# Who makes the low halves of the first layer's weights: VectorE or GpSimd

## The chip, the cores and the metric

One core of a Trainium2 chip runs the kernel. The metric is the device time of one execution in microseconds. TensorE, VectorE (DVE in the rows), ScalarE (ACT), GpSimd (POOL) and the DMA queue of SyncE (SP) each run their own list of instructions in order, and meet through semaphores.

## The reference

Four batches of eight heads, 768 steps, head size 48: a linear attention whose state is a matrix per head that turns and decays by a complex gate per key channel; then two MLP layers over 3072 tokens of width 384 with 2048 hidden units. The first has a leaky ReLU, the second an ELU.

```python
for t in range(S):
    new_re = ar * S_re - ai * S_im          # ar, ai: gate of step t, clipped to 0.999
    new_im = ar * S_im + ai * S_re
    S_re, S_im = new_re + outer(k[t], v[t]), new_im
    y[t] = q[t] @ S_re
h = x @ w_in;  g = maximum(0.01 * h, h);                 x = g @ w_out      # layer 1
h = x @ w_in2; g = where(h > 0, h, exp(minimum(h, 0)) - 1); out = g @ w_out2 # layer 2
```

## The kernel before

The attention is done in 24 chunks of 128 steps (6 per batch, batches interleaved). The first MLP layer starts on the first two chunks while the later ones are still computed; its seven tiles have 2, 3, 4, 4, 4, 4 and 3 chunks. The second layer has six tiles of 512 tokens. Each tile is 16 items: `up(n)` (L866) multiplies the tile by one strip of `w_in` of 128 hidden units, the activation is made by ScalarE (L366) and VectorE (L562), and `down(n)` (L886) multiplies by the strip of `w_out`.

Every matrix product of the MLP is made of three: a float32 operand is split in a high half, rounded to `fp32r`, and a low half, the rest. TensorE adds hi x hi, hi x lo and lo x hi. For the weights this split is made once per layer and strip. A strip is 128 x 768 numbers: 384 columns of `w_in` and 384 of `w_out`. There are 16 strips per layer (`FC`), n = 0 to 15 for the first. SyncE loads strip n into one of two raw buffers `wraw` (`WS = 2`) with four DMAs (L275, L279); ScalarE casts it to the high half (L356, semaphore `w_hi`); VectorE subtracts the high half from the raw strip (L553, semaphore `w_lo`). The load of strip n waits for the low half of strip n - 2 to be done, since it reuses that raw buffer. `up(n)` of the first tile waits for the low half of strip n.

The order of work on each engine is one loop over numbered slots, `for a in SLOTS`. In each slot an engine issues what falls due there: items of the MLP every 64 slots, steps of attention chunks every 256, and for the first eight chunks and the first layer's 16 strips the slots that are written out as lists. `weights_at(a, 0, lead)` gives the strips of the first layer whose entry in the list `lead` equals `a`, and those of the second layer by a formula. Since every engine takes its list in order, an instruction that waits holds up all behind it on that engine.

Steps of a chunk that the text names:
- L603, L604, L608, L412 to L418, L623: squares, their sum, the gain of the gate. L898 on TensorE turns the gain over to channels; L632 is its running product, L918 turns it back.
- L616 to L618, L433: the angle. L906 sums angles on TensorE for the first chunks; L658 to L660 bring the sum into one turn (L650 is a running sum for the later ones).
- L451 to L455, L467 to L470 on ScalarE: roots, sines and cosines. L679 to L683 scale q and k on VectorE, L706 and L707 turn them. L948 turns them over to channels on TensorE, L483 copies them out on ScalarE, L956 makes the scores, L714 masks them, L971 and L980 make y, L491 and L746 split y into the high and low half of x.
- L571 is the low half of the activation.

GpSimd makes constants at the start, masks and an identity, and then has no work.

Of the kernel before, what the change touches and what calls it, by code (L numbers as in the profile page):

```python
# [6 lines left out]
F32 = mybir.dt.float32  # L7
F32R = mybir.dt.float32r
ALU = mybir.AluOpType
# [16 lines left out]
def fused(nc, sem, q, k, v, a_re, a_im, weights, out, hidden, weak, attention, mlps):  # L26
# [9 lines left out]
    KC, FC = E // P, F // P  # L36
    FIRST, START, PACE, LEAD = -100122, 848, 64, 8
    WLAG, XSTEP, WS, TB = 3, 4, 2, TOK // P
# [16 lines left out]
    def chunks_at(a, offset, lead=()):  # L55
        m, r = divmod(a - START - offset, 4 * PACE)
        return [c for c, x in enumerate(lead) if x == a] + ([m + LEAD] if r == 0 and 0 <= m < M - LEAD else [])
# [5 lines left out]
    def first(m):  # L63
        return m < B

    def end(m):
        return m >= M - B
# [7 lines left out]
    with ExitStack() as ctx:  # L75
        def sb(name, shape, dt=F32):
            return ctx.enter_context(nc.sbuf_tensor(name, shape, dt))
# [4 lines left out]
        ws = [sb(f"w_{n}", [P, FC, 2, E], F32R) for n in ("hi", "lo")]  # L82
        wraw = sb("wraw", [P, WS, 2, E])
# [107 lines left out]
        w_hi, w_lo = sem("w_hi"), sem("w_lo")  # L191
# [19 lines left out]
        def weights_at(a, ahead, lead):  # L211
            j, r = divmod(a + ahead - PACE * ((T1 - 1) * FC + WLAG), PACE)
            return [i for i, x in enumerate(lead) if x == a] + ([FC + j] if r == 0 and 0 <= j < FC else [])
# [326 lines left out]
        def _(dve):  # L540
# [57 lines left out]
            def square_sum(m):  # L598
                x = sq_of(m)
                if m < 2:  # L600
                    dve.wait_ge(in_re[m], 16)
                    dve.wait_ge(in_im[m], 16)
                    step(vec.tensor_tensor(x, gate[:, m], gate[:, m], ALU.mult))  # L603
                    vec.scalar_tensor_tensor(x[:, 0], x[:, 0], 0.0, x[:, 1], ALU.add, ALU.add,  # L604
                                             accum_out=sizes[:, m:m + 1]).then_inc(sq_sum, 1)
                else:
                    dve.wait_ge(squares, m - 1)
                    vec.tensor_tensor(x[:, 0], x[:, 0], x[:, 1], ALU.add).then_inc(sq_sum, 1)  # L608
# [100 lines left out]
            def mask(m):  # L709
                if used(m):  # L710
                    dve.wait_ge(y_made, used(m))
                for half, bank in enumerate(halves(m)):
                    dve.wait_ge(scores_made, 2 * m + half + 1)
                    vec.tensor_tensor(scm_of(m)[:, 4 * half:4 * half + 4], split(bank[:], 4),  # L714
                                      causal[:].unsqueeze(1).broadcast_to([P, 4, P]), ALU.mult).then_inc(masked, 1)
# [41 lines left out]
            def verdict():  # L757
                dve.wait_ge(worst_t, 1)
                vec.tensor_reduce(worstrow[:, 0:1], chain[0:1, 0:2 * P], mybir.AxisListType.X, ALU.min)
                step(vec.tensor_reduce(worstrow[:, 1:2], chain[0:1, 2 * P:2 * P + D2], mybir.AxisListType.X, ALU.min))  # L760
                step(vec.tensor_scalar(worstrow[:, 1:2], worstrow[:, 1:2], WEAK, None, ALU.is_ge))
                step(vec.tensor_tensor(flags[:], worstrow[:, 0:1], worstrow[:, 1:2], ALU.mult))
                vec.tensor_scalar(weak[:], flags[:], 0.5, None, ALU.is_lt).then_inc(judged, 1)

            dve.wait_ge(const_ready, 10)
            for a in SLOTS:
                if a == JUDGE + 2 * PACE:
                    verdict()
                for m in chunks_at(a, 864, (-136, -136, -71, 147, 498, 765, 1204, 1396)):
                    mask(m)  # L770
                for m in chunks_at(a, 292, (-451, -451, -298, -171, -109, 51, 456, 781)):
                    square_sum(m)
                for m in chunks_at(a, 377, (-393, -349, -240, -128, -9, 181, 569, 834)):
                    gains(m)
                for m in chunks_at(a, 663, (-205, -157, -135, -32, 279, 659, 915, 1252)):
                    ends_out(m)
                for m in chunks_at(a, 976, (-138, -115, -17, 301, 564, 899, 1233, 1438)):
                    if not end(m):
                        sum_state(m)
                if (n := item_at(a, 18)) is not None:  # L780
                    split_g(n)
                if a == JUDGE:
                    judge()
                for m in chunks_at(a, 545, (-307, -291, -204, -109, 92, 402, 712, 1122)):
                    phases(m)
                if (T := finished_at(a)) is not None:
                    if T < len(tiles) - 1:
                        result(T)
                    else:
                        last_result()  # L790
                for m in chunks_at(a, 440, (-362, -324, -211, -119, 14, 359, 697, 1036)):
                    decays(m)
                for m in chunks_at(a, 1053, (-100122, -100056, -100001, -99969, 594, 1013, 1356, 1592)):
                    if not first(m) and not end(m):
                        next_state(m)
                for m in chunks_at(a, 367, (-450, -368, -283, -200, -75, 162, 453, 867)):
                    tangents(m)
                for m in chunks_at(a, 697, (-214, -200, -129, 13, 250, 682, 991, 1315)):
                    turns(m)
                if (x := x_step_at(a)) is not None:  # L800
                    split_x(*x)
                for n in weights_at(a, 0, (-326, -210, -169, -168, -122, -36, 47, 73, 246, 249, 380, 414, 516, 530, 703, 752)):
                    split_w(n)
                for m in chunks_at(a, 562, (-216, -215, -159, -61, 232, 509, 795, 1230)):
                    scale_by_decay(m)
                for m in chunks_at(a, 985, (-121, -120, 31, 296, 666, 890, 1282, 1530)):
                    chunk_to_x(m)
                for m in chunks_at(a, 602, (-306, -290, -185, -48, 206, 443, 828, 1231)):
                    ends(m)
                if (n := item_at(a, 82)) is not None:  # L810
                    from_h(n)
# [8 lines left out]
        @block.gpsimd  # L820
        def _(pool):
            gp = nc.gpsimd
            gp.memset(vs[:, 0], 0.0)
            gp.memset(vs[:, 1], 0.0).then_inc(pads_ready, 1)
            gp.memset(ident[:], 0.0).then_inc(pool_chain, 1)
            gp.memset(causal[:], 1.0).then_inc(pool_chain, 1)
            gp.memset(pick[:], 0.0).then_inc(pool_chain, 1)
            gp.memset(member[:], 1.0).then_inc(pool_chain, 1)
            pool.wait_ge(pool_chain, 4)
            gp.affine_select(out=ident[:], in_=ident[:], compare_op=ALU.not_equal, fill=1.0, base=0,  # L830
                             pattern=[[-1, P]], channel_multiplier=1).then_inc(const_ready, 1)
            gp.affine_select(out=causal[:], in_=causal[:], compare_op=ALU.is_ge, fill=0.0, base=0,
                             pattern=[[1, P]], channel_multiplier=-1).then_inc(const_ready, 1)
            gp.affine_select(out=member[:, 0], in_=member[:, 0], compare_op=ALU.is_ge, fill=0.0, base=D - 1,
                             pattern=[[0, HP]], channel_multiplier=-1).then_inc(const_ready, 1)
            gp.affine_select(out=member[:, 1], in_=member[:, 1], compare_op=ALU.is_ge, fill=0.0, base=-D,
                             pattern=[[0, HP]], channel_multiplier=1).then_inc(const_ready, 1)
            gp.affine_select(out=pick[:], in_=pick[:], compare_op=ALU.not_equal, fill=-0.5, base=0,
                             pattern=[[0, 2], [-1, D]], channel_multiplier=1).then_inc(pool_chain, 1)
            pool.wait_ge(pool_chain, 5)  # L840
            gp.affine_select(out=pick[:], in_=pick[:], compare_op=ALU.not_equal, fill=-0.5, base=-D,
                             pattern=[[0, 2], [-1, D]], channel_multiplier=1).then_inc(const_ready, 1)
            gp.memset(ones[:], 1.0).then_inc(const_ready, 1)
            gp.memset(lneps[:], math.log(MAG_EPS)).then_inc(const_ready, 1)
            gp.memset(half[:], -0.5).then_inc(const_ready, 1)
            gp.memset(rest[:], 0.75).then_inc(const_ready, 1)
            gp.memset(endmin[:], 1.0).then_inc(const_ready, 1)


        @block.tensor  # L850
# [605 lines left out]
```

## Time and profile before

| what | value |
|---|---|
| median of three runs | 1046.76 us (1046.31 to 1048.47) |
| profiled execution, its own time | 1047.74 us |
| its span | 1046.0 us |
| TensorE busy | 1010.8 us (97%), 6926 matmuls |
| VectorE busy | 680.1 us (65%) |
| ScalarE busy | 575.9 us (55%) |
| GpSimd busy | 3.2 us, 21 instructions |
| DMA | 51.57 MB, mean 49 GB/s |

The span is what the trace covers; the time of an execution holds a little more around it. Busy shares over the whole span hide that the first tenth is another kind of work than the rest, so the windows by stage say more than this table. Matmul ends are modelled in the trace.

### The profile page before, as it was taken

To read this page: it belongs to the slowest core of one execution; us is meant where nothing else is said; L and a number is where in the kernel's file an instruction comes from. 1 tells how busy PE (TensorE), PEld (TensorE's weight loads), DVE (VectorE), ACT (ScalarE), POOL (GpSimd) and SP (SyncE) were. 2 spreads that over 40 slices of the span, in tenths; PEclk is the share of its full clock that TensorE was granted. 3 is DMA by queue.
4 is the path that set the end of the run, shared out by engine and by line. 5 is a ranking of instruction groups with operands and counts; after the bars stand their busy time and mean duration, and the time that the engine had idled before them with its cause. 6 is when DMAs were issued, how large, how long until landed. Compare 5 with 4: busy or idle time off the path is not lost.

```text
span 1046.0 us, 17995 instructions
## 1 busy us (share of the span) xinstructions
PE 1010.8 (97%) x6926; PEld 907.4 (87%) x6926; DVE 680.1 (65%) x1361; ACT 575.9 (55%) x1089; POOL 3.2 (0%) x21
## 2 busy tenths in 40 slices
PE   2889999999999999999999999999999999999998
PEld 1779999988888888888888999999999999999997
DVE  7999988887777777777753376445445444454443
ACT  8988877776666667666643365323333233333332
POOL 1000000000000000000000000000000000000000
PEclk8899999999999999999999999999999999999999
DMA  7564343222222232223200244001010010010000
GB/s 151 105 121 101 70 54 78 45 39 39 61 39 39 39 69 39 38 40 76 54 1 1 79 133 144 1 1 61 1 53 9 1 61 1 16 46 1 31 1 34
DMA packets 176044, 51.57 MB, mean 49 GB/s; under 512 B 151504, under 2 KB 172112, under 8 KB 175952
## 3 DMA queue, kind: packets, MB, share of 16 engines
q1 hardware_dynamic: 175952, 50.35, 22.4%
q8 instruction: 57, 0.93, 0.4%
q14 instruction: 35, 0.29, 0.1%
HBM read 40.89 MB, written 9.44 MB: 48 GB/s over the span
## 4 chain that ended last, share of the span: by engine, by line
PE 91%; DVE 5%; issue 1%; ACT 1%; DMA 1%; SPq 0%; ACTq 0%; DVEq 0%
PE ph L866 37%; PE acc L886 33%; PE even L886 5%; PE odd L996 2%; PE even L948 2%; PE odd L948 2%; PE even L956 2%; PE odd L956 2%; PE even L971 1%; PE chain L898 1%; PE even L980 1%; PE even L975 1%; PE even L984 1%; PE chain L918 1%; DMA wraw<-in_moe_w_out 1%
## 5 line engine op out<-in xcount | busy, mean ns | idle before, releaser
L374 ACT CAST g_hi<-gf 128x512 fp32r<-128x512 f32 (+2 forms) x208 | 122.4, 588 | 219.0 <-PE even L886 128.9
L866 PE MATMUL ph<-x_hi,w_lo 128*128 128x512 f32 (+2 forms) x624 | 235.1, 377 | 0.0
L866 PE MATMUL ph<-x_lo,w_hi 128*128 128x512 f32 (+2 forms) x624 | 234.6, 376 | 0.0
L866 PE MATMUL ph<-x_hi,w_hi 128*128 128x512 f32 (+2 forms) x624 | 233.6, 374 | 0.0
L366 ACT ACTIVATE gx<-ph 128x512 f32<-128x512 f32 (+2 forms) x208 | 117.8, 566 | 157.2 <-PE ph L866 156.7
L571 DVE TENSOR_TENSOR g_lo<-gf,g_hi 128x512 fp32r<-128x512 f32 (+2 forms) x208 | 134.6, 647 | 105.3 <-ACT g_hi L374 104.1
L866 PEld LDWEIGHTS ph<-x_hi,w_lo 128*128 128x128 f32 x624 | 117.6, 188 | 19.2
L866 PEld LDWEIGHTS ph<-x_lo,w_hi 128*128 128x128 f32 x624 | 117.7, 189 | 16.8
L866 PEld LDWEIGHTS ph<-x_hi,w_hi 128*128 128x128 f32 x624 | 117.8, 189 | 16.2
L886 PE MATMUL acc<-g_hi,w_hi 128*128 128x512 f32 (+2 forms) x336 | 128.8, 383 | 0.3 <-DVE g_lo L571 0.2
L886 PE MATMUL acc<-g_hi,w_lo 128*128 128x512 f32 (+2 forms) x336 | 121.3, 361 | 0.0
L886 PE MATMUL acc<-g_lo,w_hi 128*128 128x512 f32 (+2 forms) x336 | 120.9, 360 | 0.0
L564 DVE TENSOR_SCALAR gx<-gx 128x512 f32<-128x512 f32 x96 | 41.1, 428 | 121.1 <-ACT gx L366 121.1
L886 PE MATMUL acc<-w_lo,g_hi 128*128 128x384 f32 x288 | 97.5, 338 | 0.0
L886 PE MATMUL acc<-w_hi,g_hi 128*128 128x384 f32 x288 | 97.2, 338 | 0.0
L886 PE MATMUL acc<-w_hi,g_lo 128*128 128x384 f32 x288 | 96.9, 336 | 0.0
L562 DVE TENSOR_TENSOR gf<-ph,gx 128x512 f32<-128x512 f32 (+2 forms) x112 | 68.0, 607 | 19.9 <-ACT gx L366 19.8
L886 PEld LDWEIGHTS acc<-g_hi,w_lo 128*128 128x128 f32 x336 | 63.1, 188 | 8.3
L886 PEld LDWEIGHTS acc<-g_hi,w_hi 128*128 128x128 f32 x336 | 63.4, 189 | 7.3 <-issue 0.8
L886 PEld LDWEIGHTS acc<-g_lo,w_hi 128*128 128x128 f32 x336 | 63.5, 189 | 5.9
L566 DVE SCALAR_TENSOR_TENSOR gf<-ph,gx 128x512 f32<-128x512 f32 x96 | 66.4, 692 | 3.3
L348 ACT ACT_TABLE_LOAD x49 | 62.9, 1283 | 1.6 <-PEq L1446 0.8
(216 smaller groups left out, 1541.3 us busy)
## 6 DMA issues: line engine op xcount, KB each, us to landing
wraw<-in_moe_w_out SPq DMA_DIRECT2D x32, 192.0 KB
gate<-in_a_re SPq DMA_DIRECT2D x24, 192.0 KB, 4.1
gate<-in_a_im SPq DMA_DIRECT2D x24, 192.0 KB, 4.1
qk<-in_q SPq DMA_DIRECT2D x24, 192.0 KB, 3.1
qk<-in_k SPq DMA_DIRECT2D x24, 192.0 KB, 3.7
rot<-hidden SPq DMA_DIRECT2D x6, 768.0 KB, 5.8
out<-res SPq DMA_DIRECT2D x5, 768.0 KB, 4.3
wraw<-in_moe_w_in SPq DMA_DIRECT2D x48, 64.0 KB
```

The lines of the kernel that those rows point to most:

```text
L348: act.preload_act_table_set(name)
L366: sc.activation(gx[:, n % 2, 0:size], ph[n % 2][:, 0:size], ACT.Exp if layer else ACT.Copy, scale=1.0 if layer else 0.01).then_inc(h_act, 1)
L374: sc.copy(gs[0][:, n % 2, 0:size], gf[:, n % 2, 0:size]).then_inc(g_hi, 1)
L562: vec.tensor_tensor(fb, hb, xb, ALU.max).then_inc(g_full, 1)
L564: vec.tensor_scalar(xb, xb, 1.0, -1.0, ALU.min, ALU.add).then_inc(e_ready, 1)
L566: vec.scalar_tensor_tensor(fb, hb, 0.0, xb, ALU.max, ALU.add).then_inc(g_full, 1)
L571: vec.tensor_tensor(gs[1][:, n % 2, 0:size], gf[:, n % 2, 0:size], gs[0][:, n % 2, 0:size].bitcast(F32), ALU.subtract).then_inc(g_lo, 1)
L866: ins = mm(ph[n % 2][:, 0:size], ws[hi][:, j, 0, kc * P:(kc + 1) * P], xs[lo][:, T % 2, kc, 0:size], start=i == 0, stop=i == KC * len(PART ...
L886: ins = mm(o, lhs, rhs, start=j == 0 and i == 0, stop=j == FC - 1 and i == 2)
L948: ins = tr(bank[0:D2, h * P:(h + 1) * P], rot[:, i, 4 * half + h].rearrange("p r d -> p (r d)"), ident[:])
L956: ins = mm(bank[:, (h % 4) * P:(h % 4 + 1) * P], k_of(m)[:, h], q_of(m)[:, h], start=True, stop=True)
L996: ins = mm(sum_bank(m)[0:D2, h * DP:(h + 1) * DP], rot[:, 1, h].rearrange("p r d -> p (r d)"), vs[:, m % 2, h], start=True, stop=True)
```

## The change

The list of slots for the first layer's strips on VectorE becomes empty, so VectorE makes low halves only for the second layer. GpSimd, behind its constants, loops over the 16 strips of the first layer, waits for each high half and makes the low half by the same subtraction into the same tile. The casts on ScalarE, the loads on SyncE with their slots, and TensorE's waits are as they were.

```diff
@@ VectorE @@
-                for n in weights_at(a, 0, (-326, -210, -169, -168, -122, -36, 47, 73, 246, 249, 380, 414, 516, 530, 703, 752)):
+                for n in weights_at(a, 0, ()):
                     split_w(n)
@@ GpSimd @@
             gp.memset(endmin[:], 1.0).then_inc(const_ready, 1)
+            for n in range(FC):
+                pool.wait_ge(w_hi, n + 1)
+                gp.tensor_tensor(ws[1][:, n], wraw[:, n % WS], ws[0][:, n].bitcast(F32), ALU.subtract).then_inc(w_lo, 1)
```

## Rows read from the trace of the kernel before

**Rows 1.** Windows: start, end, length, each engine's busy us, PEclk, DMA share, GB/s.

```profile
10.00:50.00 40.00, 25.27 (x217) 21.59 (x218) 37.20 (x85) 37.42 (x70) 0.00 (x0) 0.83 0.70 131
50.00:84.00 34.00, 28.48 (x275) 26.00 (x274) 31.45 (x74) 29.59 (x61) 0.00 (x0) 0.95 0.56 109
84.00:125.00 41.00, 40.20 (x443) 39.19 (x443) 39.22 (x90) 35.77 (x77) 0.00 (x0) 1.00 0.45 102
125.00:440.00 315.00, 315.00 (x2567) 280.32 (x2566) 251.39 (x547) 225.14 (x445) 0.00 (x0) 1.00 0.29 48
```

**Rows 2.** Waits of TensorE from 84 us on: total us, times, longest.

```profile
PE chain L929 <- DVE qk L683: 0.5, 1, 0.5
PE acc L886 <- DVE g_lo L571: 0.2, 1, 0.2
```

**Rows 3.** Groups by line, first 130 us: count, busy us, mean ns, idle before.

```profile
L553 DVE TENSOR_TENSOR w_lo<-wraw,w_hi 128x768 fp32r<-128x768 f32 x16 | 15.0, 946 | 0.6 <-ACT w_hi L356 0.5
```

**Rows 4.** Timeline of VectorE: start us, duration us, instruction, idle before it.

```profile
5.05 0.96 DVE L603 TENSOR_TENSOR sq<-gate 128x768 f32<-128x768 f32 x1 [5.05 <-DMA gate<-in_a_im]
...
13.14 0.53 DVE L623 SCALAR_TENSOR_TENSOR res<-res 128x384 f32<-128x384 f32 x1
...
14.86 1.36 DVE L632 TENSOR_TENSOR_SCAN gx<-acc,ones 96x128 f32<-96x128 f32 x4 [0.31 <-PE acc L898]
...
18.90 0.55 DVE L608 TENSOR_TENSOR sq<-sq 128x384 f32<-128x384 f32 x1
...
29.63 0.95 DVE L707 TENSOR_TENSOR rot<-roots,qk 128x768 f32<-128x768 f32 x1
...
33.89 0.56 DVE L658 TENSOR_SCALAR turn<-chain 128x384 f32<-128x384 f32 x1 [1.05 <-PE chain L906]
...
39.70 1.81 DVE L553 TENSOR_TENSOR w_lo<-wraw,w_hi 128x768 fp32r<-128x768 f32 x2
41.44 0.55 DVE L679 TENSOR_TENSOR sines<-chain,sines 128x384 f32<-128x384 f32 x1
...
47.35 0.94 DVE L706 SCALAR_TENSOR_TENSOR rot<-sines,qk 128x768 f32<-128x768 f32 x1
...
55.49 0.56 DVE L658 TENSOR_SCALAR turn<-chain 128x384 f32<-128x384 f32 x1 [1.75 <-PE chain L906]
...
117.38 0.95 DVE L553 TENSOR_TENSOR w_lo<-wraw,w_hi 128x768 fp32r<-128x768 f32 x1
```

**Rows 5.** Timeline of ScalarE: casts of strips 0, 1 and 15, and one L470.

```profile
11.81 0.81 ACT L356 CAST w_hi<-wraw 128x768 fp32r<-128x768 f32 x1
...
27.97 0.82 ACT L356 CAST w_hi<-wraw 128x768 fp32r<-128x768 f32 x1
...
46.33 0.51 ACT L470 ACTIVATE sines<-sines 128x384 f32<-128x384 f32 x1
...
115.45 0.84 ACT L356 CAST w_hi<-wraw 128x768 fp32r<-128x768 f32 x1
```

**Rows 6.** Timeline of GpSimd: three pairs of neighbours.

```profile
0.80 0.52 POOL L823 MEMSET vs<- 128x512 f32 x1 [0.29 <-POOLq L1446]
1.26 0.52 POOL L824 MEMSET vs<- 128x512 f32 x1
1.73 0.20 POOL L825 MEMSET ident<- 128x128 f32 x1
1.87 0.20 POOL L826 MEMSET causal<- 128x128 f32 x1
...
2.46 0.29 POOL L830 TENSOR_SCALAR_AFFINE_SELECT ident<-ident 128x128 f32<-128x128 f32 x1 [0.23 <-POOL member L828]
2.71 0.29 POOL L832 TENSOR_SCALAR_AFFINE_SELECT causal<-causal 128x128 f32<-128x128 f32 x1
```

**Rows 7.** Waits of SyncE's queue, first 125 us: total us, times, longest.

```profile
SPq L275 <- DVE w_lo L553: 28.3, 6, 7.8
```

**Rows 8.** Timeline of TensorE: the first matmul of `up(15)` in the first tile.

```profile
119.02 0.29 PE L866 MATMUL ph<-x_hi,w_hi 128*128 128x256 f32 x1
```

## Prediction

> **What bounds the kernel now.** I read the windows by stage first. From 125 us on TensorE is busy without a gap at full clock (315 of 315 us), and from 84 to 125 us nearly so; before that it is busy 25.3 of 40 us (10 to 50) and 28.5 of 34 us (50 to 84), at a mean granted clock of 0.83 and 0.95 (part of it at 1.2 in place of 2.4 GHz) [rows 1]. The reader should see that only the first 84 us have TensorE time to win or lose in bulk. TensorE's waits after 84 us say the same: two waits, 0.7 us in total, both on VectorE [rows 2]. In those first 84 us two engines are nearly full: VectorE 37.2 of 40 and 31.5 of 34 us, ScalarE 37.4 of 40 and 29.6 of 34 us [rows 1]. The order on every engine is written out by hand and fixed, so whoever is late there makes TensorE late, and a delay at 84 us is a delay of the end. The timelines of VectorE and ScalarE are read next, around the slots of the strips.
>
> **What leaves VectorE.** The 16 subtractions that make the low halves of the first layer's strips: 16 x 0.946 us busy = 15.1 us, all within the first 130 us [rows 3]. Two in a row take 1.81 us, less an overlap of 0.07 at the next start; from start to start one takes 0.87 us (39.70 for two, and the next instruction at 41.44) [rows 4]. I use 0.87. Ten of the 16 (strips 0 to 9) run before 84 us, the last one at 117.38 [rows 4]. The code of the second layer's 16 is as it was.
>
> What those ten are worth, if nothing else changes:
> - Strips 0 and 1 give nothing. Behind the first one VectorE still waits 0.31 us for TensorE, whose transpose needs the L623 at 13.14, ahead of the subtraction; behind the second it waits 1.05 us for the cumulative sum of the angles [rows 4].
> - Strips 2 and 3 (39.70) free 1.74 us, but the L706 at 47.35 needs ScalarE's L470, which starts at 46.33 and ends at 46.84 [rows 4, 5]. So 0.5 us is left.
> - Strip 4 gives 0.8 us more: the low halves of x come right behind it, then TensorE's transposes and first layer product, and the 1.75 us that VectorE waits at 55.49 is for them, so it moves along [rows 4]. That is 1.3 us.
> - Strips 5 to 9 give some 0.2 us in all: there the scaling steps wait for ScalarE's roots, or VectorE for TensorE. Total at 84 us: 1.5 us.
> - Behind 84 us TensorE can win back at most its 0.7 us of idle [rows 2]. The total is -2.2 us. Its bounds are 0 and 8 x 0.87 = 7.0 us; ScalarE's idle time from 50 to 84 us, 34 - 29.6 = 4.4 us [rows 1], makes more than about 4.5 us implausible.
>
> **What arrives on GpSimd.** 16 subtractions 128x768 with two inputs in SBUF. The trace has no such instruction on GpSimd. From start to start a MEMSET of 512 columns takes 0.46 us and one of 128 takes 0.14 us, so 0.83 ns per column written; an AFFINE_SELECT (one input) of 128 columns takes 0.25 us, some 1.7 ns per column [rows 6]. For 768 columns that is 0.64 us from the one, 1.35 us from the other; with a second input read at 0.83 ns per column 2.0 us. Ends: 0.7 and 2.0 us. I take 1.7 us, by the AFFINE_SELECT, which also reads, plus part of the second input. In a sentence that the sum does not need: the Trainium skill (GPSIMD Engine Reference, "Elementwise — side-by-side cycle accounting") gives 4497 ns for a two-input operation on 2048 columns, by which an estimate for 768 is 1.7 us; no row here shows it.
>
> GpSimd's queue holds nothing else once its 21 small instructions are over (3.2 us busy; none from 10 us on [rows 1]), so nothing stands behind a waiting subtraction. It starts when the high half is there, so the low half comes about 1.8 us after ScalarE's cast ends. Before, VectorE came to strip 15 at 117.38 on a cast that ended at 116.29 [rows 4, 5], and SyncE's 28.3 us of waiting for low halves [rows 7] shows that others came later still, so most low halves now come earlier. The buffers get free earlier too. Earlier loads win little, since TensorE has only the 0.7 us to win behind 84 us. No load, cast or matmul is added or moved in its queue.
>
> **The disputed cost: two engines reading SBUF together.** After the change GpSimd works 16 x 1.7 = 27 us inside a stretch where VectorE is full. The trace shows no overlap of the two: GpSimd is busy 3.2 us at the very start and never from 10 us on, and VectorE's first instruction starts at 5.05, behind a DMA [rows 1, 4]. What a row shows is that VectorE reads two SBUF operands at once: the L608 with two SBUF inputs takes 0.55 us for 384 columns, and the L658 with one input in PSUM 0.56 us [rows 4]. Bounds: the two engines do not disturb each other (0), or one stands still for the whole instruction of the other whenever both want two SBUF operands. With the hold, by strips:
> - Strip 0: the cast (11.81, 0.81) ends at 12.62 [rows 5]; GpSimd runs from 12.7 to 14.4. The scan before 13.2 reads one SBUF operand and goes on; the L623 of 13.14 waits to 14.4: +1.3 us. TensorE's idle transpose and the scan at 14.86 follow it [rows 4].
> - Strip 1: the cast (27.97, 0.82) ends at 28.79 [rows 5], when VectorE is in the first of the two rotations (L706, L707), both with two SBUF inputs. The second, at 29.63, waits: +1.7 us. TensorE waits for it. Subtotal +3.0 us.
> - Strips 2 and 3 (their casts move with the delay so far): the first falls on a scan and a wait for TensorE, 0; the second takes about 1.2 us out of the 1.74 freed, net -0.5 us. Subtotal +2.5 us.
> - Strips 4 to 9: one (strip 7) falls on a scan. Five holds of 1.7 = 8.5 us against six removed instructions of 0.87 = 5.2 us: +3.3 us. Together +5.8 us.
> - Some of it lands where ScalarE is last (strips 5 to 9 above, where time won by VectorE gave almost nothing); I take off 0.8 us. Total +5.0 us.
> - Strips 10 to 15 at 0: six holds of 1.7 = 10.2 us at most, of which some six tenths meet two-input work, against 5.2 us removed and 1.8 us of idle (41 - 39.2) [rows 1].
>
> With a GpSimd instruction of 1.35 us the same steps give 0.9 + 1.35 - 0.9 + 1.6 = +3.0 us, with 2.0 us +8 us. I cannot choose between hold and no hold by rows; the choice is a judgement. For the hold speaks that VectorE uses two SBUF reads a cycle and that the added work needs two as well. By the Trainium skill (SBUF — State Buffer, "Who interferes with whom") a VectorE instruction with two SBUF inputs contends with a GpSimd instruction that reads SBUF, and the one that comes second is blocked until the first is done: by that rule +5.0 us, without it -2.2 us; no row of this trace shows which.
>
> **Forecast and rivals**, against the median of 1046.76 us. The profiled execution's own time is 1047.74 us (span 1046.0), 1.0 us above the median, so 1052.7 us by that execution is 1051.8 us by the median. The measurement tells about 0.2% (2.1 us) from no change.
> - **Forecast: hold.** GpSimd's reads stop VectorE's two-input instructions in the first 84 us: +5.0 us, 1051.8 us; own range 1049.5 to 1055. Chance 0.52.
> - **Rival 1: no disturbance.** VectorE is relieved and ScalarE takes over as the bound: -2.2 us, 1044.6 us (1043 to 1046). Chance 0.32. For it: GpSimd is empty and the slack of every strip is there. Against it: nothing in the trace has both engines at work. It decides if VectorE's instructions keep their durations beside GpSimd's.
> - **Rival 2: partial.** Either instruction is only stretched, or GpSimd is the one that waits most of the time. The break-even is where a strip's subtraction costs VectorE as much as it frees: 0.87 us for strips 2 to 9, and nothing for 0 and 1. With half of each hold, 0.65 + 0.85 - 1.1 + (4.25 - 5.2) = -0.5 us: 1046.2 us. Chance 0.13.
> - **Rival 3: low halves too late.** The last strip is the tightest: cast 115.45 + 0.84 = 116.29, low half by GpSimd at 118.1, by VectorE at 118.3 before; TensorE wants it at 119.02 [rows 4, 5, 8]. Only with over 2.6 us per instruction would it wait, and then by tenths: 1047.5 us. Chance 0.03.
>
> Chances: faster by over 0.2% 0.18 (a little over half of rival 1), within 0.2% 0.29, slower 0.53. Range: from rival 1's 1044.0 to 1054.5 us, which leaves out the lowest part of rival 1 and the top of the hold.
>
> **What would show it.** The profile after has 16 subtractions on POOL of 1.3 to 2 us from the cast's end, no L553 on VectorE in the first 125 us. If the hold is right, VectorE's two-input forms (L623, L707, L618, L682) have single instructions of 1.5 to 2.5 us in the first 120 us, or idle gaps in front of them beside a GpSimd instruction, and VectorE's L623 for chunk 1 ends near 15 us instead of 13.7. TensorE's last product with strip 15 in the first tile, now at 119.02 [rows 8], comes 5 us later. If those durations are as before and that product comes 2 us earlier, rival 1 is right. The prediction is wrong if the two engines read side by side, or if GpSimd's instruction is much longer than 2 us.

## The result: 12 us slower

The changed kernel takes 1059.66 us (median of five, 1057.57 to 1061.35); the kernel before took 1048.47 us on the same chip (1046.31 to 1049.33). The ratio, taken from the means of the two sets of five, is 1.0114, 95% interval 1.0093 to 1.0134; so the loss is 11.2 us by the medians and 11.9 us by the means. The direction was forecast, the size was not: 1051.8 us with a range to 1054.5 us stood on record. The profiled execution took 1059.66 us; its span is 1057.9 us, 11.9 us over the span of 1046.0 us before.

The timeline of GpSimd in the changed kernel has the 16 subtractions, each started by ScalarE's cast. Four of them:

```profile
12.90 1.80 POOL L850 TENSOR_TENSOR w_lo<-wraw,w_hi 128x768 fp32r<-128x768 f32 x1 [8.71 <-ACT w_hi L356]
30.30 2.51 POOL L850 TENSOR_TENSOR w_lo<-wraw,w_hi 128x768 fp32r<-128x768 f32 x1 [15.60 <-ACT w_hi L356]
...
51.04 1.85 POOL L850 TENSOR_TENSOR w_lo<-wraw,w_hi 128x768 fp32r<-128x768 f32 x1 [6.22 <-ACT w_hi L356]
...
69.39 3.59 POOL L850 TENSOR_TENSOR w_lo<-wraw,w_hi 128x768 fp32r<-128x768 f32 x1 [7.29 <-ACT w_hi L356]
```

One takes 1.80 us where it runs at once, against VectorE's 0.946 us [rows 3], and the slowest, 3.59 us, had to wait itself. The answer to rows 4 is in the timeline of VectorE. Every line but the L632 is an instruction that took 0.16 to 0.95 us before:

```profile
13.30 1.81 DVE L623 SCALAR_TENSOR_TENSOR res<-res 128x384 f32<-128x384 f32 x1
16.30 1.36 DVE L632 TENSOR_TENSOR_SCAN gx<-acc,ones 96x128 f32<-96x128 f32 x4 [1.18 <-PE acc L901]
...
31.07 2.56 DVE L707 TENSOR_TENSOR rot<-roots,qk 128x768 f32<-128x768 f32 x1
...
43.54 1.69 DVE L680 SCALAR_TENSOR_TENSOR sines<-sines,roots 128x384 f32<-128x384 f32 x1
...
51.15 2.56 DVE L707 TENSOR_TENSOR rot<-roots,qk 128x768 f32<-128x768 f32 x1
...
60.44 2.08 DVE L618 SCALAR_TENSOR_TENSOR ang<-inv,ang 128x384 f32<-128x384 f32 x1
...
75.90 1.86 DVE L659 TENSOR_SCALAR turn<-turn 128x384 f32<-128x384 f32 x1
...
82.89 1.88 DVE L623 SCALAR_TENSOR_TENSOR sq<-sq 128x384 f32<-128x384 f32 x1
...
85.14 1.74 DVE L671 SCALAR_TENSOR_TENSOR endmag<-rootd,parted 96x8 f32<-96x8 f32 x1
...
98.50 1.87 DVE L571 TENSOR_TENSOR g_lo<-gf,g_hi 128x256 fp32r<-128x256 f32 x1 [0.35 <-ACT g_hi L374]
...
102.34 1.95 DVE L659 TENSOR_SCALAR turn<-turn 128x384 f32<-128x384 f32 x1
...
107.13 2.19 DVE L618 SCALAR_TENSOR_TENSOR ang<-inv,ang 128x384 f32<-128x384 f32 x1
...
127.62 2.03 DVE L571 TENSOR_TENSOR g_lo<-gf,g_hi 128x256 fp32r<-128x256 f32 x1
```

Read two timelines side by side here. The L623 at 13.30 starts while GpSimd's first subtraction runs (12.90 to 14.70) and ends 0.4 us after it. The L632 is a scan with no GpSimd instruction beside it; it keeps its 1.36 us and only comes late, behind TensorE. The L671 handles 8 columns, took 0.16 us before and takes 1.74 us: the time is not the instruction's own, it ends when GpSimd does. The other 12 instructions and the L623 at 116.07 (0.89 us) are longer by 18.2 us in all than the same instructions in the kernel before, by 0.35 to 1.63 us each; what was taken off VectorE is 16 x 0.87 = 13.9 us. Instructions with an operand in PSUM kept their times: L679 (it reads `chain`) and L562 (it reads `ph`) beside GpSimd at 42.96 and 82.56 took 0.55 and 0.42 us, as before.

The windows of the changed kernel, with the stretches of [rows 1], and after them TensorE from the first matmul of `up(6)` to that of `up(16)`, first after, then before (in a fence of its own):

```profile
10.00:50.00 40.00, 23.69 (x178) 20.82 (x182) 35.35 (x78) 34.39 (x66) 7.93 (x4) 0.79 0.67 126
50.00:84.00 34.00, 26.99 (x297) 24.61 (x286) 32.14 (x63) 29.82 (x62) 11.23 (x5) 0.95 0.59 114
84.00:125.00 41.00, 34.88 (x326) 34.11 (x325) 34.38 (x68) 29.00 (x61) 11.31 (x7) 0.92 0.42 99
125.00:440.00 315.00, 314.36 (x2643) 280.80 (x2642) 253.35 (x551) 225.44 (x447) 2.04 (x1) 1.00 0.30 49
92.55:136.46 43.91, 40.77 (x433) 39.66 (x432) 38.88 (x82) 34.38 (x73) 11.19 (x6) 0.95 0.37 77
```

```profile
84.97:124.61 39.64, 38.84 (x434) 37.83 (x433) 37.86 (x88) 34.41 (x75) 0.00 (x0) 1.00 0.47 106
```

`up(6)` starts at 92.55 in place of 84.97 (+7.6 us), `up(16)` at 136.46 in place of 124.61 (+11.9 us), and the span is 11.9 us longer: nothing more is lost or won behind it. So 7.6 us come from the stage that the forecast had at +5.0, and 4.3 us from the stage that it had at 0. In that last stage TensorE's idle time went from 0.8 to 3.1 us, and its busy time for the same work from 38.8 to 40.8 us, at a mean granted clock of 0.95 in place of 1.00. Of TensorE's waits from 10 to 140 us in the changed kernel these five grew most, all on what the held instructions make or pass on (GpSimd's loop moves TensorE's lines by three: L901 is L898 of the kernel before, L932 is L929, L951 is L948, L889 is L886). Before, in this order, they were 12.8, 1.6, 1.8, 2.1 and 0.2 us:

```profile
PE chain L901 <- DVE sq L623: 14.7, 3, 10.7
PE chain L932 <- DVE qk L683: 3.6, 1, 3.6
PE even L951 <- DVE rot L707: 3.4, 1, 3.4
PE acc L901 <- DVE res L623: 3.4, 1, 3.4
PE acc L889 <- DVE g_lo L571: 3.1, 3, 2.2
```

### The profile page after: what moved, and what is told of

Its sections match the earlier page's. It is cut to its first block, busy times and chain, and to the rows that moved or that the text cites. A ratio compares the mean times of both kernels' runs of the same rounds, so it can differ in the third digit from the quotient of the medians.

```text
span 1057.9 us, 17995 instructions
## 1 busy us (share of the span) xinstructions
PE 1013.6 (96%) x6926; PEld 910.9 (86%) x6926; DVE 685.1 (65%) x1345; ACT 576.0 (54%) x1089; POOL 35.7 (3%) x37
## 4 chain that ended last, share of the span: by engine, by line
PE 91%; DVE 5%; ACT 2%; issue 1%; DMA 0%; SPq 0%; DVEq 0%; ACTq 0%
PE ph L869 37%; PE acc L889 33%; PE even L889 5%; PE odd L999 2%; PE even L951 2%; PE odd L951 2%; PE even L959 2%; PE odd L959 2%; PE even L974 1%; PE chain L901 1%; PE even L983 1%; PE even L978 1%; PE even L987 1%; PE chain L932 1%; PE chain L921 1%
## 5 line engine op out<-in xcount | busy, mean ns | idle before, releaser
L571 DVE TENSOR_TENSOR g_lo<-gf,g_hi 128x512 fp32r<-128x512 f32 (+2 forms) x208 | 137.6, 662 | 105.3 <-ACT g_hi L374 104.1
L889 PE MATMUL acc<-g_hi,w_hi 128*128 128x512 f32 (+2 forms) x336 | 129.9, 387 | 3.1 <-DVE g_lo L571 3.1
L889 PE MATMUL acc<-g_hi,w_lo 128*128 128x512 f32 (+2 forms) x336 | 122.5, 365 | 0.0
L889 PE MATMUL acc<-g_lo,w_hi 128*128 128x512 f32 (+2 forms) x336 | 122.0, 363 | 0.0
L889 PE MATMUL acc<-w_lo,g_hi 128*128 128x384 f32 x288 | 97.5, 338 | 0.0
L889 PE MATMUL acc<-w_hi,g_hi 128*128 128x384 f32 x288 | 97.2, 338 | 0.0
L889 PE MATMUL acc<-w_hi,g_lo 128*128 128x384 f32 x288 | 96.9, 336 | 0.0
L562 DVE TENSOR_TENSOR gf<-ph,gx 128x512 f32<-128x512 f32 (+2 forms) x112 | 68.0, 608 | 19.3 <-ACT gx L366 19.3
L889 PEld LDWEIGHTS acc<-g_hi,w_hi 128*128 128x128 f32 x336 | 64.5, 192 | 10.4 <-DVE g_lo L571 3.8
L889 PEld LDWEIGHTS acc<-g_hi,w_lo 128*128 128x128 f32 x336 | 64.4, 192 | 8.3
L889 PEld LDWEIGHTS acc<-g_lo,w_hi 128*128 128x128 f32 x336 | 64.6, 192 | 5.9
```

Source lines behind the costliest of these rows:

```text
L562: vec.tensor_tensor(fb, hb, xb, ALU.max).then_inc(g_full, 1)
L571: vec.tensor_tensor(gs[1][:, n % 2, 0:size], gf[:, n % 2, 0:size], gs[0][:, n % 2, 0:size].bitcast(F32), ALU.subtract).then_inc(g_lo, 1)
L889: ins = mm(o, lhs, rhs, start=j == 0 and i == 0, stop=j == FC - 1 and i == 2)
```

## The experiments

**Is it GpSimd's reading?** Two theories: A, GpSimd's reads of SBUF stop VectorE; C, nothing is stopped, but low halves and loads come at other times and upset the hand-written order. In the first kernel GpSimd only writes (a MEMSET to zero; the first layer's low halves are left out):

```diff
-                gp.tensor_tensor(ws[1][:, n], wraw[:, n % WS], ws[0][:, n].bitcast(F32), ALU.subtract).then_inc(w_lo, 1)
+                gp.memset(ws[1][:, n].bitcast(F32), 0.0).then_inc(w_lo, 1)
```

> GpSimd's 16 instructions of the first layer only write: each sets its strip's low half to zero (128x768, no input), at the same place and behind the same waits, so the low halves of the first layer are left out of the result. Theory A (GpSimd's reads stop VectorE's instructions): nothing is read, so L623 of chunk 1 is back at 0.53 us, L707 at 0.95 us, and only the relief is left: 2 us faster than the kernel before, 1045 us. Theory B (any GpSimd instruction that touches SBUF stops VectorE, writes too): each holds for its own 0.7 us, about +2 us. Theory C (the order of the queues is upset once VectorE is not the one that makes low halves, whatever GpSimd does): still some +8 to +12 us.

Measured: 1043.71 us against 1046.72 us, ratio 0.9971 (0.9962 to 0.9981): 3.0 us faster. GpSimd's first MEMSET runs beside the same L623 that was held before, and the L623 does not mind. Timelines of GpSimd and VectorE in this kernel:

```profile
12.81 0.74 POOL L850 MEMSET w_lo<- 128x768 f32 x1 [8.61 <-ACT w_hi L356]
...
68.84 0.74 POOL L850 MEMSET w_lo<- 128x768 f32 x1 [3.91 <-ACT w_hi L356]
```

```profile
13.27 0.53 DVE L623 SCALAR_TENSOR_TENSOR res<-res 128x384 f32<-128x384 f32 x1
...
69.02 0.77 DVE L658 TENSOR_SCALAR turn<-phase 128x384 f32<-128x384 f32 x1
```

So C is wrong where it says that the loss comes with the move itself, and the relief is real: 3.0 us. The second line of VectorE is the one exception among the instructions beside a MEMSET: a one-input instruction from SBUF to SBUF that takes 0.36 us elsewhere took 0.77 us beside a MEMSET.

In the second kernel the work is only added: VectorE keeps all its subtractions, GpSimd repeats those of strips 0 to 13.

```diff
+                    sp.wait_ge(p_lo, min(n - WS + 1, FC - 2))       # SyncE, load n
+                if n == FC - 1:                                     # VectorE, split_w
+                    dve.wait_ge(p_lo, FC - 2)
+            for n in range(FC - 2):                                 # GpSimd
+                pool.wait_ge(w_hi, n + 1)
+                pool.wait_ge(p_lo, n)
+                gp.tensor_tensor(ws[1][:, FC - 1], wraw[:, n % WS], ws[0][:, n].bitcast(F32), ALU.subtract).then_inc(p_lo, 1)
```

> VectorE makes all low halves as in the kernel before; GpSimd makes those of strips 0 to 13 a second time, at the times of the changed kernel, into the place of strip 15's low half, which VectorE overwrites at the end. Work is only added, none taken away, and no low half is late. Theory A (reads hold VectorE): fourteen holds of 1.8 us with no relief; the loss is that of the changed kernel or more, +11 to +18 us, with instructions of 1.7 to 2.6 us on VectorE. Theory C (lateness or order, no hold): within 1 us of the kernel before.

Measured: 1063.98 us against 1046.72 us, ratio 1.0172 (1.0155 to 1.0189): +17.3 us. GpSimd's added work costs this much, with VectorE's own work and order as before. A raw buffer is also held until GpSimd has read it, but in this trace no cast of the first layer waits for its load. The loss is about what the changed kernel lost plus the relief that it got (12 + 3 = 15 us). VectorE's own subtractions have two SBUF inputs too, and two of the 16 are held (2.57 and 2.59 us in place of 0.95). All that is longer on VectorE sums to 15.4 us, not more than the 18.2 us of the changed kernel, so where the 2 us above 15 come from stays open.

**Which strips?** Strips 0 to 9 by GpSimd and the rest by VectorE in the old slots, and the other way about (the list of slots with `None` for GpSimd's strips, GpSimd's loop over its own, and a wait on `w_lo` where one engine follows the other).

```diff
-                for n in weights_at(a, 0, ()):
+                for n in weights_at(a, 0, (None, None, None, None, None, None, None, None, None, None, 380, 414, 516, 530, 703, 752)):
-            for n in range(FC):
+            for n in (0, 1, 2, 3, 4, 5, 6, 7, 8, 9):
                 pool.wait_ge(w_hi, n + 1)
+                pool.wait_ge(w_lo, n)
```

> Strips 0 to 9 by GpSimd, 10 to 15 by VectorE in their old slots. The stage up to 84 us of the kernel before is as in the changed kernel, that behind it has no hold. If the forecast's split were right, all the loss is here: +12 us. If the holds of strips 10 to 15 cost as the trace of the changed kernel says (the delay grows from 6.4 us at the L683 of 82.65 to 11.7 us at that of 122.09), this one loses 6 to 8 us.

> Strips 0 to 9 by VectorE in their old slots, 10 to 15 by GpSimd. If late strips cost nothing, as the forecast said (six holds against the removed work and VectorE's idle time): within 1 us of the kernel before. If their holds fall on instructions that TensorE waits for (L571, L618): +3 to +5 us, and the sum of this one and of the one with strips 0 to 9 is about the changed kernel's +11 us.

Measured: strips 0 to 9 cost 1056.02 us, ratio 1.0085 (1.0063 to 1.0106), +9.3 us by the medians; strips 10 to 15 cost 1050.48 us, ratio 1.0039 (1.0025 to 1.0053), +3.8 us. The sum of 13 us is the changed kernel's loss within the intervals. Six late strips, expected to be covered, are a quarter to a third of the loss. Their mechanism shows in TensorE's waits from 84 to 140 us of the kernel with strips 10 to 15, where before there were 0.2 us on L571 [rows 2] (L573 is L571 and L892 is L886 in the lines of this kernel):

```profile
PE acc L892 <- DVE g_lo L573: 3.4, 3, 2.2
```

**How much of it is the second input, how much the length?** GpSimd copies the raw strip (one input; the low halves hold the raw weights), and GpSimd subtracts in four pieces of 192 columns:

```diff
+                gp.tensor_copy(ws[1][:, n], wraw[:, n % WS]).then_inc(w_lo, 1)
```

```diff
+                for i in range(4):
+                    s = slice(i % 2 * 192, i % 2 * 192 + 192)
+                    ins = gp.tensor_tensor(ws[1][:, n, i // 2, s], wraw[:, n % WS, i // 2, s],
+                                           ws[0][:, n, i // 2, s].bitcast(F32), ALU.subtract)
+                ins.then_inc(w_lo, 1)
```

> GpSimd's 16 instructions copy the raw strip into the low half's place: one SBUF input in place of two, so the low halves of the first layer hold the raw weights and the result is not the reference's. If one reading input is enough to stop VectorE, the holds are as long as this instruction runs, which by the MASK instructions (1.7 ns a column) is up to 1.35 us and by the MEMSET (0.74 us measured for 768 columns) 0.8 us: between 0 and +6 us, with single L623, L707 or L618 instructions lengthened by about that duration. If only a second input stops it: as with the MEMSET, -3 us and all durations as before.

> Each of GpSimd's subtractions in four pieces of 192 columns. If an instruction holds VectorE until it ends, a piece of about 0.5 us does so for 0.5 us, and VectorE's next instruction comes in between pieces, or doesn't where the next piece stands ready. If VectorE gets its turn between pieces, the same total of held time is spread, more of it falls beside instructions that do not mind, and low halves come later: +5 to +8 us. If GpSimd keeps its turn through all four, as the changed kernel: +11 us or a little more.

Measured: the copy 1048.48 us, ratio 1.0015 (1.0006 to 1.0025), the pieces 1050.85 us, ratio 1.0040 (1.0025 to 1.0055). The copy takes 0.83 us and holds VectorE for up to 0.64 us, 5.5 us in all: one input is enough, and the hold shrinks with the instruction (up to 1.63 us by the subtraction of 1.80 us). With pieces the L707 is held once for a piece; the timeline of VectorE:

```profile
29.78 1.34 DVE L707 TENSOR_TENSOR rot<-roots,qk 128x768 f32<-128x768 f32 x1
```

That is +0.4 us in place of +1.6 us. VectorE gets its turn between pieces, the sum of the lengthened instructions falls from 18.2 to 8.2 us, and the loss from 12 to about 4 us. It went a little better than the +5 to +8 us expected.

**Can the clash be placed away?** The changed kernel with 13 subtractions each behind a step of VectorE that is followed by instructions without a second SBUF input:

```diff
+            behind = {0: (gain_ready, 2), 1: (turned, 1), 3: (scaled, 3), 4: (gain_ready, 4), 5: (tan_ready, 5),
+                      6: (turned, 4), 7: (g_lo, 3), 8: (g_lo, 5), 9: (turned, 5), 10: (g_lo, 7), 12: (g_lo, 9),
+                      14: (g_lo, 12), 15: (g_lo, 13)}
             for n in range(FC):
+                if n in behind:
+                    pool.wait_ge(*behind[n])
                 pool.wait_ge(w_hi, n + 1)
```

> The changed kernel with 13 of GpSimd's 16 subtractions behind one more wait, on a step of VectorE after which it has 1.3 to 4 us of instructions with at most one SBUF input (scans, masks, products with PSUM) or waits: strips 0 and 4 behind L623, 1, 6 and 9 behind L707, 3 behind L683, 5 behind L618, 7, 8, 10, 12, 14 and 15 behind an L571. Strips 2, 11 and 13 start as before. Theory A: most holds vanish and the relief stays: 2 to 3 us faster than the kernel before (1044 to 1045 us), with one or two lengthened VectorE instructions left. If time is lost because low halves and loads are late, this one, whose low halves come later still, is slower than the changed kernel: over +11 us.

Measured: 1048.01 us, ratio 1.0012 (1.0003 to 1.0021). Eleven microseconds are won back by waiting longer, which settles it against lateness as the cause of the loss. It is 1.3 us slower than the kernel before, so the forecast gain of 2 to 3 us was missed: six VectorE instructions are still longer, by 6.2 us. Three of them:

```profile
90.44 1.69 DVE L644 COPY carry<-turn 128x3 f32<-128x3 f32 x1
...
93.69 1.87 DVE L659 TENSOR_SCALAR turn<-turn 128x384 f32<-128x384 f32 x1
...
105.12 2.07 DVE L623 SCALAR_TENSOR_TENSOR sq<-sq 128x384 f32<-128x384 f32 x1
```

A copy of three columns and the scalar operation L659 read one SBUF operand only. I had taken both for harmless. Next, those strips went back to VectorE: nine strips on GpSimd (0, 1, 3 to 9), then seven (0, 1, 3 to 7), with their steps from the list above.

```diff
-                for n in weights_at(a, 0, ()):
+                for n in weights_at(a, 0, (None, None, -169, None, None, None, None, None, None, None, 380, 414, 516, 530, 703, 752)):
-            for n in range(FC):
+            for n in (0, 1, 3, 4, 5, 6, 7, 8, 9):
```

> Strips 0, 1 and 3 to 9 by GpSimd, each behind the step of VectorE that it had in the kernel with 13 placed strips; strip 2 and strips 10 to 15 by VectorE in their old slots. In the kernel with placed strips the long VectorE instructions left were L659 at 34.5 (+0.75 us), L571 at 86.4 (+0.7 us) and three beside strips 10, 11 and 13 (L644, L659, L623, +1.5 us each). The last three and the first are gone here. If VectorE is only held by what runs beside a GpSimd read, the relief before 84 us shows: 1.0 to 2.5 us faster than the kernel before. If that relief is worth nothing without the one behind 84 us: within 1 us.

> As the one with nine strips on GpSimd, but strips 8 and 9 also go back to VectorE. No hold on L571 near 86 us is left. The relief of strips 8 and 9 falls where VectorE then waits for ScalarE's sines, so it should cost nothing to give it up: 1.0 to 2.5 us faster than the kernel before, equal to the nine strips within 0.7 us.

Measured: nine strips 1048.17 us (1045.33 to 1050.29), ratio 1.0013 (1.0004 to 1.0022); seven strips 1046.11 us (1045.04 to 1050.50), ratio 1.0000 (0.9991 to 1.0009). The holds are gone (0.8 and 0.1 us left), the forecast gain of 1.0 to 2.5 us is not there by the medians, and the executions spread over 5 us. The profiled execution of the seven strips is one of the long ones, 1049.03 us. In its timeline of ScalarE, a cast waits for its raw strip:

```profile
69.10 0.83 ACT L356 CAST w_hi<-wraw 128x768 fp32r<-128x768 f32 x1 [1.24 <-DMA wraw<-in_moe_w_out]
```

TensorE waits for what is queued behind that cast on ScalarE. Its longest wait from 60 to 80 us, and its windows around (busy 1.50 us of 4 in the pause and 3.54 us of 4 behind it, where the granted clock is 0.65):

```profile
PE even L957 <- ACT qd L483: 2.8, 1, 2.8
```

```profile
66.00:70.00 4.00, 1.50 (x11) 1.14 (x11) 3.90 (x11) 2.71 (x6) 0.70 (x1) 1.00 0.53 141
70.00:74.00 4.00, 3.54 (x19) 3.44 (x20) 1.07 (x3) 3.90 (x11) 1.83 (x1) 0.65 0.17 53
```

With VectorE relieved, SyncE's list is next: the load of strip 7 stands behind three loads of v and goes out at 64.17 us. In the nine strips' profiled execution, one of the short ones (1045.64 us), it goes out at 62.94 us and the cast does not wait. Three kernels with that load one place earlier:

```diff
-                for n in weights_at(a, PACE, (-167, -141, -112, 18, 26, 43, 87, 150, 150, 168, 212, 219, 239, 267, 300, 307)):
+                for n in weights_at(a, PACE, (-167, -141, -112, 18, 26, 43, 87, 121, 150, 168, 212, 219, 239, 267, 300, 307)):
```

> The nine placed strips, and SyncE's load of strip 7 one place earlier in its list, ahead of the loads of v for chunk 4 (slot 121 in place of 150). In the seven strips' trace that load went out at 64.2 us and ScalarE waited 1.24 us for it, then TensorE 2.8 us for ScalarE, and its clock fell (0.65 in that stretch); in the nine strips' trace it went out at 62.9 us and nothing waited. If this late load is what takes the relief away in most executions: 1044.5 to 1045.5 us with little spread, against 1048.2 us and a spread from 1045.3 to 1050.3. If the spread has another cause: as before, about 1048 us.

> The seven placed strips with the same earlier load of strip 7. If the late load is the cause: 1044.5 to 1045.5 us, against 1046.1 us (1045.0 to 1050.5) without. If not: no change.

> The kernel before with the same earlier load of strip 7 and nothing else. There VectorE makes strip 5's low half at 63.35, so the load can't go out before 64.3 us wherever it stands in the list, and the loads of v now wait behind it: within 1 us of the kernel before, rather slower. Faster by over 2 us would mean that the load's place alone is worth something and GpSimd's part nothing.

Measured: nine strips 1045.80 us (1045.34 to 1048.23), ratio 0.9992 (0.9983 to 1.0001); seven strips 1044.73 us (1044.05 to 1045.82), ratio 0.9980 (0.9971 to 0.9989); the kernel before with the earlier load 1047.73 us, ratio 1.0005 (0.9996 to 1.0014); the kernel before 1047.30 us. The seven strips land in the range expected, the nine strips 0.3 us above it. Seven placed strips with one moved load beat the kernel before by 2.6 us, which is 0.2%, and the spread went from 5.5 us without the moved load to 1.8 us; strip 7's cast comes at 68.01 us and does not wait. The load alone shows no gain, and neither does GpSimd's part without it.

## Why the prediction was right in direction and wrong in size

- **What bounds the kernel: right in part.** All of the loss is there before `up(16)`; behind it both spans run in step. But the sentence that only the first 84 us have TensorE time to lose in bulk was wrong: 4.3 us were lost behind them.
- **What leaves VectorE, -2.2 us: right in kind, somewhat low.** The kernel that has the relief without reads gained 3.0 us. Behind `up(6)` it gained more than the 0.7 us that were called the most to win: from there to `up(16)` it took 38.2 us in place of 39.6 us.
- **What arrives, 1.7 us each: right.** 1.80 us where it runs at once, 0.1 us after the cast. The Trainium skill (GPSIMD Engine Reference, "Elementwise — side-by-side cycle accounting") has GpSimd about twice as slow as VectorE for two inputs; here it is 1.80 to 0.946 us, 1.9 times.
- **The hold: right.** The choice was a judgement that the rows left open, and it fell on the true side. Strip 0 was forecast at +1.3 us and its L623 is 1.3 us longer (0.53 to 1.81); strip 1 at +1.7 us, its L707 1.6 us longer; strip 3 at 1.2 us, its L680 1.1 us. The Trainium skill (SBUF — State Buffer, "Who interferes with whom") has two-input VectorE instructions contend with GpSimd's reads, not with its writes, and VectorE's faster two-port forms with both: the traces agree, with L623 held 1.3 us by the subtraction and unchanged by the MEMSET, and L658, which takes 0.36 us from SBUF and 0.56 us from PSUM, 0.4 us longer beside the MEMSET.
- **Strips 0 to 9, +5.0 us: mis-sized.** At `up(6)` the delay was 7.6 us, and the kernel with these strips alone lost 9.3 us by the medians. The holds themselves are 11.5 us (eight instructions), against the 12.7 us of the forecast's steps (1.3 + 1.7 + 1.2 + 8.5). What was too good is the other side: I set 5.2 us of removed instructions against the holds of strips 4 to 9 in full, though the same text had found that strips 5 to 9 give only 0.2 us when removed, because others end last there. And 0.8 us was taken off on top. That five of strips 4 to 9 hold something came out by luck: strip 7 was called harmless because it falls on a scan, but its subtraction came at 75.60 on the L658 right behind the scan and held the L659 (+1.5 us), while strip 6 held nothing.
- **Strips 10 to 15 at 0: this step failed.** It weighed holds against removed work and idle time as sums over the stage. The kernel with these strips alone lost 3.8 us. A hold is 1.6 us in one piece, and two of them hit L571, which makes the low half of the activation that TensorE multiplies next; TensorE had 0.2 us of idle on it before [rows 2], so there is no cover of that size at that place, and the 0.87 us that is freed elsewhere doesn't help it. TensorE idled 3.1 us in place of 0.8.
- **A term that was missing: the clock, worth less than it looks.** TensorE worked 1.4 us of the 5 us from 85 and 3.0 us of the 5 us from 105, and in the 5 us behind each (from 90 and from 110) its mean granted clock was 0.66. So the same matmuls from `up(6)` to `up(16)` took 40.8 in place of 38.8 us. Yet not all of these 2 us were lost. The kernel with strips 10 to 15 alone on GpSimd has the same five instructions held (7.2 us in all, against 6.6 us) and full clock between the same two points (the lines are below this list). It took 43.0 us, 3.4 us more than before, against 4.3 us more in the changed kernel. So by these two traces the lower clock cost about 0.9 us there; the rest of the longer matmuls took the place of idle time (3.9 us idle here, 3.1 us there). No run sets the clock alone.
- **The time before has such a fall of the clock, too.** In its profiled execution the mean granted clock is 0.95 from 50 to 84 us [rows 1]. The kernel with strips 10 to 15 on GpSimd runs the same instructions up to there, at full clock in its trace. It reaches `up(6)` at 83.81, 1.2 us earlier than the 84.97 us of before. Measured from there, strips 0 to 9 cost 8.7 us in the changed kernel, nearer to the 9.3 us that they cost alone; the forecast's +5.0 us was off by more than the windows of one trace say.
- **Rivals 1 and 2 (no disturbance, partial): refuted.** Thirteen instructions on VectorE are longer by 0.35 to 1.63 us, 18.2 us in all, which is more than the 13.9 us taken off.
- **Rival 3 (late low halves): refuted.** Later low halves, in the placed kernel, made it faster by 11 us.

Windows of the kernel with strips 10 to 15 on GpSimd, from 50 to 84 us and from the first matmul of its `up(6)` to that of its `up(16)`:

```profile
50.00:84.00 34.00, 28.40 (x286) 26.00 (x287) 33.04 (x76) 31.04 (x64) 0.00 (x0) 1.00 0.57 110
83.81:126.83 43.02, 39.09 (x434) 37.87 (x432) 40.36 (x83) 35.02 (x75) 11.19 (x6) 1.00 0.44 97
```

## What to carry to other kernels

In these runs work moved from VectorE to GpSimd came back as holds, mostly of VectorE and now and then of GpSimd itself, where GpSimd read SBUF and VectorE had an instruction with two SBUF inputs, or a one-input one from SBUF to SBUF. Count a hold of VectorE as a block of up to the GpSimd instruction's whole length at the place where it falls, and ask what waits for that one instruction; sums of holds, savings and idle time over a stage gave 0 here for what cost 3.8 us. If the work must move, two things each won most of the loss back: starting a piece behind a VectorE step that is followed by scans or PSUM operands (from +12 to +1.3 us), and cutting it in pieces (to +4 us). Neither alone beat the kernel before, and both together were not tried. Then look which queue is late next.

## What was not expected of the hardware

- One-input instructions are held as well where they go from SBUF to SBUF: L659 (0.36 us alone) took 1.86 and 1.95 us, and in the placed kernel the three-column copy L644 (0.16 us alone) took 1.69 us.
- GpSimd isn't always next when it waits. At 69.39 its subtraction took 3.59 us in place of 1.80: VectorE's L706 (69.47) and L707 (70.33) both ran at their usual 0.95 us first, while at 31.07 it was the L707 that had to wait, behind an L706 that ran undisturbed. No run shows what decides it.
- The same kernel's executions differ by several microseconds: 1045.3 to 1050.3 us with nine placed strips, and 1045.3 to 1048.2 us with one load moved by one place. That the margin between a load and its cast, about a microsecond, decides which it is was read from two traces and not shown for the others. The times also go with the granted clock of the execution: with nine strips 1050.1 and 1050.3 us at a mean of 0.989, and 1045.3 and 1045.6 us at 1.000; in the kernel before, run beside the last three kernels, 1048.9 and 1049.3 us at 0.989, and 1046.2 us at 1.000. Whether the clock is a cause of it or only follows the waits isn't shown.
